# Expert tiles loaded one tile sooner, control numbers read later, the even tail put next to the loop

## The reference

```python
for s in range(S):
    fresh_e = int(np.argmax(logits[b, s]))
    if s == 0 or local_gate[b, s] < 0.5:
        e = fresh_e
    else:
        e = prev_e if prev_e >= 0 else fresh_e
    prev_e = e
    ...
    h = np.maximum(x[b, s] @ w1[e], 0.0)
    out[b, s] = p[e] * (h @ w2[e])
```

## Time and profile before

| | us |
|---|---|
| median of 3 runs | 699.01 |
| the runs | 695.54 to 708.86 |
| profiled execution, time | 697.34 |
| profiled execution, span | 695.5 |
| PE busy | 653.3 (94%) |
| VectorE busy | 319.5 (46%) |
| ScalarE busy | 207.7 (30%) |
| GpSimd busy | 213.2 (31%) |

### The profile page before, as it was taken

How to read it: one execution, slowest core, us unless ns; L and a number is a source line. 1 busy time by engine, 2 the same in 40 slices (tenths; PEclk the granted TensorE clock), 3 DMA queues, 4 the chain that set the end, 5 groups by cost and what they waited for, 6 DMA issues and landing times.

```text
span 695.5 us, 10536 instructions
## 1 busy us (share of the span) xinstructions
PE 653.3 (94%) x3370; PEld 530.5 (76%) x3371; DVE 319.5 (46%) x831; ACT 207.7 (30%) x410; POOL 213.2 (31%) x119
## 2 busy tenths in 40 slices
PE   8999999578989998999979989999999999999997
PEld 6777878456877787877767658888888888888886
DVE  4999787477435434534525775432231112311112
ACT  3666544204232332344202653132211112111110
POOL 0000002037567767799313745352000000000000
PEclk9999999879999999999999999999999999999999
DMA  8655356137447547578234322310010000000001
GB/s 304 249 208 177 115 172 247 43 122 257 155 161 261 182 167 256 180 221 283 90 139 121 91 91 91 122 61 1 1 60 1 1 0 1 30 32 1 0 1 60
DMA packets 35267, 82.66 MB, mean 119 GB/s; under 512 B 3347, under 2 KB 7699, under 8 KB 35221
## 3 DMA queue, kind: packets, MB, share of 16 engines
q1 hardware_dynamic: 17808, 40.20, 16.3%
q10 hardware_dynamic: 15492, 35.56, 15.5%
q0 software_dynamic: 1920, 6.29, 2.8%
HBM read 67.09 MB, written 14.94 MB: 118 GB/s over the span
## 4 chain that ended last, share of the span: by engine, by line
PE 76%; DVE 10%; DMA 7%; issue 4%; SPq 1%; ACT 1%; DVEq 0%; POOL 0%; ACTq 0%; POOLq 0%
PE psum L597 20%; PE psum L599 19%; PE psum L598 19%; DMA xs<-x_sorted 5%; PE psum L1886 5%; PE psum L1858 3%; PE psum L1869 2%; PE psum L1977 2%; PE psum L1796 1%; PE psum L1994 1%; PE psum L2037 1%; DVE prob L1405 1%; DMA bounds_i<-in_n_local 1%; DVE prob_t L1419 1%; DVE ys L1587 1%
## 5 line engine op out<-in xcount | busy, mean ns | idle before, releaser
L722 POOL TENSOR_TENSOR w<-raw,w 128x1024 fp32r<-128x1024 f32 x56 | 132.4, 2400 | 49.6 <-ACT w L820 49.6
L1750 DVE SCALAR_TENSOR_TENSOR act_t<-psum,act_t 128x512 fp32r<-128x512 f32 x48 | 33.2, 691 | 191.6 <-ACT act_t L1101 191.6
L820 ACT ACTIVATE w<-raw 128x1024 fp32r<-128x1024 f32 x64 | 67.4, 1058 | 132.9 <-PE psum L599 66.2
L1101 ACT ACTIVATE act_t<-psum 128x512 fp32r<-128x512 f32 x48 | 28.7, 598 | 217.8 <-PE psum L599 217.8
L597 PE MATMUL psum<-un_t,wc 128*128 128x512 f32 x192 | 75.3, 392 | 1.4 <-DVE un_t L1674 1.4
L597 PE MATMUL psum<-wc,act_t 128*128 128x512 f32 x192 | 75.6, 394 | 0.0
L598 PE MATMUL psum<-un_t,wc 128*128 128x512 f32 x192 | 75.4, 393 | 0.0
L599 PE MATMUL psum<-un_t,wc 128*128 128x512 f32 x192 | 75.4, 393 | 0.0
L599 PE MATMUL psum<-wc,act_t 128*128 128x512 f32 x192 | 74.8, 390 | 0.0
L598 PE MATMUL psum<-wc,act_t 128*128 128x512 f32 x192 | 74.8, 389 | 0.0
L874 ACT ACTIVATE prob<-prob,top 128x256 f32<-128x256 f32 (+1 forms) x96 | 46.3, 482 | 48.1 <-DVE top L1405 47.7
(11 more groups left out here) (271 smaller groups left out, 1111.3 us busy)
## 6 DMA issues: line engine op xcount, KB each, us to landing
raw<-in_moe_w ACTq DMA_DIRECT2D x60, 512.0 KB, 4.1
k_win<-in_k SPq DMA_DIRECT2D x8, 768.0 KB, 5.8
raw<-in_moe_w_ch SPq DMA_DIRECT2D x12, 512.0 KB, 3.3
v_win<-in_v SPq DMA_DIRECT2D x8, 704.0 KB, 4.6
xs<-x_sorted SPq DMA_DIRECT2D x16, 256.0 KB, 3.9
y_sorted<-ys SPq DMA_DIRECT2D x16, 256.0 KB, 2.6
q_t<-in_q SPq DMA_DIRECT2D x8, 384.0 KB, 3.4
out<-u SPq DMA_DIRECT2D x12, 256.0 KB, 2.0
```

The source lines that it names most:

```text
L722: nc.gpsimd.tensor_tensor(w[:, slot, 1, m, at_:at_ + PIECE], raw[:, n % RING, :], w[:, slot, 0, m, at_:at_ + PIECE].bitcast(f32), ALU.subt ...
L820: nc.scalar.activation(w[:, slot, 0, m, at_:at_ + PIECE], raw[:, n % RING, :], ACT.Copy).then_inc(high_done, 1)
L1101: nc.scalar.activation(act_t[n % 2][:, 0, :], bank(act_bank(n)), ACT.Relu).then_inc(act_high, 1)
L1750: nc.vector.scalar_tensor_tensor(act_t[n % 2][:, 1, :], bank(act_bank(n)), 0.0, act_t[n % 2][:, 0, :].bitcast(f32), ALU.max, ALU.subtract) ...
```

## The change

1. SyncE loads tile j+3 in step j into the other buffer, once PE has turned tile j+1. Tile 2 is asked for ahead of the loop as soon as tile 0 is turned. One tile beyond the even end is loaded and not used; ScalarE waits for it before it overwrites the region. GpSimd clears the end of `ctl` that this load's row number may be read from.
2. On PE, `place_of` is split into `ready_of` and `slot_of`. The slot of tile j+1 is read behind the transposes of hid(j), slot and readiness of tile j behind the transposes of the new tile, just ahead of the down product. The readiness of tile j+1, which wasn't used there, is not read.
3. On PE, the even tail stands in the If and the odd one in the Else. On SyncE, both share the two last steps.
4. At the start of the stage PE starts tile 0's up product before it turns tile 1, and VectorE does `share(1)` and `first_results` before tile 1's parts.
5. In the routing, the one-hot is held by expert, then tile, so that counts come out of PE in the order of the running sum. The copies `totals` and `ahead` go, for the second batch the copy of the counts as well (its counts are read from PSUM), and `area` and `count` are computed behind the slots.
6. `BANK_LAST` moves to bank 0, and four tiles' last gate sums stand before the last value product instead of two in the step before.

```diff
--- before.py
+++ after.py
@@ -232,10 +232,9 @@
     ends = rr("ends", [1, 2 * ST])
     counted = rr("counted", [P, 2 * ST * E])
     carry = rr("carry", [1, ST + 1])
-    one_hot = [rr(f"one_hot{b}", [P, ST, E]) for b in range(B)]
-    totals = rr("totals", [P, E, ST])
+    hot = [rr(f"hot{b}", [P, E, ST]) for b in range(B)]
+    one_hot = [x[:, :, :].rearrange("p e t -> p t e") for x in hot]
     upto = [rr(f"upto{b}", [P, E, ST]) for b in range(B)]
-    ahead = rr("ahead", [P, E, ST])
     area = rr("area", [P, E])
     rank = keep("rank", [P, ST, E])
     slot_f = rr("slot_f", [P, NT])
@@ -554,8 +553,9 @@
 
         small = bank(6)
         OVER = P + D
-        BANK_LOGITS, BANK_LAST, BANK_PART = (small[:, P + OVER + n * ST * (E + 1):P + OVER + (n + 1) * ST * (E + 1)]
-                                             for n in range(3))
+        BANK_LOGITS, BANK_PART = (small[:, P + OVER + n * ST * (E + 1):P + OVER + (n + 1) * ST * (E + 1)]
+                                  for n in range(2))
+        BANK_LAST = bank(0)[:, 0:ST * (E + 1)]
         BANK_FLAGS = small[0:ST, 2 * P:4 * P]
         BANK_KEEP, BANK_FRESH = small[0:ST, 2 * P:3 * P], small[0:ST, 3 * P:4 * P]
         BANK_ENDS = small[0:1, OVER:OVER + 2 * ST]
@@ -668,33 +668,32 @@
             sp.wait_ge(scattered, 16 * NT)
             for par in range(2):
                 load_tile(first_rows[par], par)
+            sp.wait_ge(xs_turned, 1)
+            load_tile(row_of(2), 0)
             sp.wait_ge(ctl_ready, 1)
             half = HALVES_LEAST + nc.sync.value_load(ctl[0:1, CTL_MORE], min_val=0, max_val=SLOTS // 2 - HALVES_LEAST)
             odd = nc.sync.value_load(ctl[0:1, CTL_ODD], min_val=0, max_val=1)
 
-            def tile_step(p, par, ahead):
+            def tile_step(p, par, loads):
 
                 j = 2 * p + par
-                if ahead >= 2:
-                    sp.wait_ge(xs_turned, j + 1)
-                    load_tile(row_of(j + 2), par)
+                if loads:
+                    sp.wait_ge(xs_turned, j + 2)
+                    load_tile(row_of(j + 3), 1 - par)
                 sp.wait_ge(ys_ready, j + 1)
                 sp.dma_start(y_sorted[ds(j * P, P), :], ys[par][:, :]).then_inc(ys_stored[par], 16)
 
             with sp.Fori(0, HALVES_LEAST - 1) as p:
-                tile_step(p, 0, 2)
-                tile_step(p, 1, 2)
+                tile_step(p, 0, True)
+                tile_step(p, 1, True)
             with sp.Fori(HALVES_LEAST - 1, SLOTS // 2 - 1) as p:
                 with nc.sync.If(half > p + 1):
-                    tile_step(p, 0, 2)
-                    tile_step(p, 1, 2)
+                    tile_step(p, 0, True)
+                    tile_step(p, 1, True)
+            tile_step(half - 1, 0, False)
+            tile_step(half - 1, 1, False)
             with nc.sync.If(odd > 0):
-                tile_step(half - 1, 0, 2)
-                tile_step(half - 1, 1, 1)
-                tile_step(half, 0, 0)
-            with nc.sync.Else():
-                tile_step(half - 1, 0, 1)
-                tile_step(half - 1, 1, 0)
+                tile_step(half, 0, False)
 
 
             for n in range(RING, 2 * FF // 256):
@@ -711,6 +710,7 @@
             nc.gpsimd.memset(ones[:, :], 1.0).then_inc(ones_ready, 1)
             for r in range(2):
                 nc.gpsimd.memset(v_flat[r][:, (2 * ST - 1) * P:], 0.0).then_inc(v_padded, 1)
+            nc.gpsimd.memset(ctl[:, CTL_ROW.stop:], 0)
             nc.gpsimd.memset(zeros[:, :], 0.0).then_inc(zeros_ready, 1)
             nc.gpsimd.memset(eps[:, :], LN_EPS).then_inc(eps_ready, 1)
 
@@ -1051,6 +1051,7 @@
             act.wait_ge(eps_ready, 1)
             scale_near(0, 0)
             scale_near(0, 1)
+            act.wait_ge(xs_loaded[0], 16 * half + 16)
             x2_part(0, 0)
             with nc.scalar.If(odd > 0):
                 last_result(2 * half + 1, 0, half)
@@ -1257,30 +1258,31 @@
             def take_counts(b):
 
                 dve.wait_ge(ranks_ready, b + 1)
-                link(nc.vector.tensor_copy(counted[:, :], BANK_COUNTED))
+                if b == 0:
+                    link(nc.vector.tensor_copy(counted[:, :], BANK_COUNTED))
 
             def rank_all(b):
-                flat_ = lambda x: x[:, :, :].rearrange("p a n -> p (a n)")
-                link(nc.vector.tensor_copy(totals[:, :, :], counted[:, ST * E:].rearrange("p (t e) -> p e t", t=ST)))
-                link(nc.vector.tensor_tensor_scan(flat_(upto[b]), row["run"], flat_(totals), 0.0, ALU.mult, ALU.add))
-                if b == B - 1:
-
-                    link(nc.vector.tensor_tensor(count[:, :], upto[0][:, :, ST - 1], upto[1][:, :, ST - 1], ALU.add))
-                link(nc.vector.tensor_tensor(ahead[:, :, :], upto[b][:, :, :], totals[:, :, :], ALU.subtract))
-                start = row["area"]
-                if b == 1:
-                    link(nc.vector.tensor_tensor(area[:, :], row["area"], upto[0][:, :, ST - 1], ALU.add))
-                    start = area[:, :]
-                link(nc.vector.tensor_tensor(ahead[:, :, :], ahead[:, :, :],
-                                             start.unsqueeze(2).broadcast_to([P, E, ST]), ALU.add))
-                link(nc.vector.tensor_tensor(rank[:, :, :], counted[:, 0:ST * E].rearrange("p (t e) -> p t e", t=ST),
-                                             ahead[:, :, :].rearrange("p e t -> p t e"), ALU.add))
+                by_tile = lambda x: x.rearrange("p (e t) -> p t e", t=ST)
+                sums_ = counted[:, :] if b == 0 else BANK_COUNTED
+                inside, totals = sums_[:, 0:ST * E], sums_[:, ST * E:]
+                start = row["area"] if b == 0 else area[:, :]
+                link(nc.vector.tensor_tensor_scan(upto[b][:, :, :].rearrange("p e t -> p (e t)"), row["run"], totals,
+                                                  0.0, ALU.mult, ALU.add))
+                link(nc.vector.tensor_tensor(rank[:, :, :], by_tile(inside),
+                                             start.unsqueeze(1).broadcast_to([P, ST, E]), ALU.add))
+                link(nc.vector.tensor_tensor(rank[:, :, :], rank[:, :, :],
+                                             upto[b][:, :, :].rearrange("p e t -> p t e"), ALU.add))
+                link(nc.vector.tensor_tensor(rank[:, :, :], rank[:, :, :], by_tile(totals), ALU.subtract))
 
             def place(b):
                 link(nc.vector.tensor_tensor(rank[:, :, :], rank[:, :, :], one_hot[b][:, :, :], ALU.mult))
                 link(nc.vector.tensor_reduce(slot_f[:, b * ST:(b + 1) * ST], rank[:, :, :], AX.X, ALU.add))
                 these = slice(b * ST, (b + 1) * ST)
                 nc.vector.tensor_copy(slots[:, these], slot_f[:, these]).then_inc(slots_ready, 1)
+                if b == 0:
+                    link(nc.vector.tensor_tensor(area[:, :], row["area"], upto[0][:, :, ST - 1], ALU.add))
+                else:
+                    link(nc.vector.tensor_tensor(count[:, :], upto[0][:, :, ST - 1], upto[1][:, :, ST - 1], ALU.add))
 
             def place_results():
 
@@ -1589,9 +1591,9 @@
                     rectify(j + 1, 1 - par, 1)
 
             x_tile(0, 0)
-            x_tile(1, 1)
             share(1)
             first_results()
+            x_tile(1, 1)
             rectify(0, 0, 0)
             rectify(0, 0, 1)
             tile_step(0, 0, 2)
@@ -1838,9 +1840,9 @@
             def rank_tokens(b):
 
                 pe.wait_ge(one_hot_ready, b + 1)
-                hot = one_hot[b][:, :, :].rearrange("p t e -> p (t e)")
-                nc.tensor.matmul(BANK_RANKS, before, hot, start=True, stop=True)
-                nc.tensor.matmul(BANK_TOTALS, ones[:, :], hot, start=True, stop=True).then_inc(ranks_ready, 1)
+                flags = hot[b][:, :, :].rearrange("p e t -> p (e t)")
+                nc.tensor.matmul(BANK_RANKS, before, flags, start=True, stop=True)
+                nc.tensor.matmul(BANK_TOTALS, ones[:, :], flags, start=True, stop=True).then_inc(ranks_ready, 1)
 
             with nc.tensor.If(windowed > 0):
 
@@ -1911,14 +1913,14 @@
                         tasks.append(lambda t=PART_STEP[n]: sum_part(t))
                     if n in THIRD_STEP:
                         tasks.append(lambda t=THIRD_STEP[n]: sum_third(t))
-                    if n == LAST_STEP:
-                        tasks += [lambda t=t: sum_last(t) for t in range(2)]
                     if n > 0:
                         values(n - 1, tasks)
+                for t in range(4):
+                    sum_last(t)
                 values(UNITS - 1)
                 pe.wait_ge(x_unit_done, UNITS)
                 turn_x(len(X_FILLS) - 1)
-                for t in range(2, ST):
+                for t in range(4, ST):
                     sum_last(t)
             with nc.tensor.Else():
                 pe.sem_inc(g_x, 1)
@@ -1994,11 +1996,11 @@
                     ins = nc.tensor.transpose(bank(4)[:, c * P:(c + 1) * P], xs[par][:, c * P:(c + 1) * P], ident)
```

(34 more changed lines are left out.)

## The result

The changed kernel takes **677.31 us** (median of 4 runs, 676.39 to 679.46), the kernel before beside it 700.1 us (4 runs, 695.54 to 708.86): ratio 0.970, 95% interval 0.9643 to 0.9757. Run again beside the last experiment it took 677.43 us (6 runs), ratio 0.9651 (0.9609 to 0.9692). The forecast was 677 with 671 to 686. Of the profiled executions the changed one took 677.65 us (span 675.8) against 697.34 (695.5), which is 19.7 us less where the sum said 20.95. All ratios here leave out runs more than 1.5% above the fastest of their own kernel; the medians take all runs.

The account below looks back on a forecast made before the run. TensorE (PE) was taken as the bound, so gains had to come from its stalls; terms of 8.1 + 2.6 + 6.1 + 3.0 + 0.75 + 0.4 = 20.95 us off 697.34 gave 676.3, predicted as 677, range 671 to 686.

Parts of the forecast that it names:

- The sum: All gains over the whole kernel added up: 20.95 us, chance 0.55 that it holds as it stands.
- Load, 8.1: Expert stage: token tile loads asked one tile sooner end PE's waits before the tile's transposes, 8.1 us.
- Control reads, 2.6: Expert stage: control reads moved behind the transposes end four issue waits at the hidden transposes, 2.6 us.
- Rival (4): Reads moved between products are bare because PE's sequencer stops running ahead after a wait: 704 us, chance 0.03.
- Against: the covered reads of odd steps: Sign against bare moved reads: in odd steps four reads are covered by matmuls already queued, no stall.
- Tail, 6.1: Behind the last loop step: without reads and long jump, PE's stall before tile 14 and slow matmuls go, 6.1 us.
- Rival (2): The tail's stall is the loop's exit, not the long jump; 2 us or more stay, 679 to 681, chance 0.15.
- Start, 3.0: Start of expert stage: sooner up product, no ReLU wait, no issue wait at tile 0, together 3.0 us.
- Slots 0.75: Routing: fewer VectorE links from counts to slots; control numbers come 0.75 us sooner.
- end of attention 0.4: End of attention: two tiles' gate sums leave the path before the last but one value product, 0.4 us.
- Expert 7's weights: GpSimd's weight pieces for expert 7: slack falls from 2.4 to 0.3 us; nothing taken, up to 1 us kept.
- Rival (1): The weights or a half-bare read give back 2 to 5 us: 679 to 682, chance 0.15.

Follow-up runs that it names:

- the last experiment: Changed kernel with the four control reads back ahead of the hidden transposes and the odd tail back next to the loop: 686.31 us.
- the second profile: Profile of the changed kernel run once more, unchanged: 676.66 us in that profile, median 677.43 us.
- experiment 11: Changed kernel with four idle control-number reads more ahead of each down product: 696.34 us, ratio 0.9912.

## Why the prediction was right, and where it wasn't

**The sum** was right within 1.3 us, in the profiled execution and by the median. What failed in it is the step that treated the terms as additive.

**Load, 8.1.** The waits went as forecast. But it isn't the worth of this edit: alone it gives 9 us by its ratio (0.013 x 703) and takes with it the head stalls, and taken out of the finished change it costs some 30 (30.6 us in the expert stage of the profile, 36 by the medians of different groups), since the other half of the change leans on it.

**Control reads, 2.6: mis-attributed.** The step was "the other four waits give 1.9 + 4 x 0.16". Those four went with the load edit. The sentence "I take nothing, as odd steps hide four" looked at steps in which no wait stood right ahead of the reads. Rival (4) named the true mechanism, "because PE's sequencer no longer runs ahead of them once it has passed a wait", and gave it 0.03 because it asked whether it holds in every step, not where a wait would stand. It holds in the steps in which the sequencer had to stand at a load's wait, at 1.2 to 1.4 us where PE was seen idle and 0.6 to 1.3 where it wasn't, and the changed kernel has none of these since the load edit took them away. "Against: the covered reads of odd steps" failed for the same reason: those reads stood a whole down product behind the wait. What the moved reads do bring, given the load edit, is 4.3 us by the medians of two groups: in the profile 2.0 at the head behind expert 7's weights and 2.0 as the reads' part of the tail.

**Tail, 6.1.** Right in size: 4.67 us before tile 14 and 1.01 of slow matmuls behind it (1.7 less 0.3 forecast; the wait at 341.25 is 0.33 and, with the overlap, 0.49 us). The long jump was taken as the price "of that order" of 2.68; it is 2.5. But the term belongs to reads and jump together, and either alone would have left 1.8. Rival (2), the loop's exit alone, is excluded as the sole cause: exit and reads without the long jump leave 1.84, exit alone nothing.
The Trainium skill ("Runtime: NRT & Kernel Launch", Instruction fetch mechanics) says that a taken branch whose target is outside the fetched window stalls for a page; the 2.5 us agree with that. Its 2048 instructions of TensorE's memory would keep a jump over some 300 inside, and the tail put back (1.76) speaks against that, unless the window is smaller than the memory, as its next remark on two lines has it.

**Start, 3.0** (measured 2.77). Right against the profile, and short by some 5 us against the usual run of before. The rows showed two operations at 1.92 and 2.32 us beside GpSimd; that these are two only by luck, and up to five in other runs, was not asked. It is the likeliest reason why the medians gained 23 and 24 us where the profiled executions gained 19.7.

**Slots 0.75 and end of attention 0.4**: 0.97 together instead of 1.15. The sums gave 0.67 (logits at 131.31), the chain to the slots 0.92 (139.83), but the control numbers only 0.37 of it: 0.2 go to the count, as forecast, and the rest is lost since a few of VectorE's small steps before them took up to 0.24 longer (143.37: 0.40 instead of 0.16). Why isn't shown; the scatter runs beside them in both kernels.

**Expert 7's weights**: slack 0.3, taken as nothing, 1 us kept. At 311.03 it was overdrawn by 0.13; in the second profile by 1.15, 1.5 with the reads put back. Rival (1) is real and stayed under its 2 us. In the second profile GpSimd's wait for ScalarE at that place is 2.30 us instead of 0.99 (301.95 against 301.05), and ScalarE had waited 4.77 instead of 3.76 us for a load of weights; why that load came later stays open.

## What to carry to other kernels

The cover of something an engine's sequencer must do is what it has queued since the last wait that held it, and such a wait need not show as idle time of the engine: look when the load landed, not only for a bracket. So before a scalar read or a jump is put down as free or as a cost, look for the wait that stands ahead of it, and take the wait away first: moved behind a wait, two cheap reads a step made the kernel 18 us slower; with the wait gone, the same move gains up to 4.
Edits that share a cover or a wait have no prices of their own. Price them as a pair, and test both the edit alone and the whole without it: alone and put back, the load edit measured 9 and some 30 us.
A kernel whose runs spread by 2% while another's spread by 0.5% may have a race for a resource in it, and one profile then shows one draw of it; several profiles, each taken of a slightly different kernel, showed 0.7 to 6.7 us for the same wait.

## What the runs showed of the hardware that I hadn't expected

- Single stalls of PE of 1.76 to 1.89 us left its clock alone (1.06 us for the eight transposes behind those at the tail). Above that the length alone does not decide: 2.17 us (load alone, 324.35), 2.43 (tail alone, 206.37), 2.73 and all from 4.26 to 6.68 lowered it to half, 2.41 (experiment 11, 358.56) and 2.71 (moved reads, 382.74) didn't. Of two stalls with only four transposes between them, 2.06 and 1.40, 0.98 and 1.18, 0.74 and 1.30 lowered it, 1.00 and 1.26 didn't. Where it fell, up to twelve products ran 0.43 us apart instead of 0.23, some 1 to 2 us more. It makes double stalls dearer than their brackets: 38 matmuls in the moved reads alone.
- A small VectorE operation in SBUF (2 to 768 numbers, twice 128x48) takes 1.9 to 2.4 us instead of 0.17 to 0.21 when it falls beside GpSimd's subtraction of 128x1024 tiles (2.36 us each), at most about the whole length of one such operation. Not each one does: L1308 (ten numbers) kept its 0.34 for two beside them. The casts and ReLUs of 128x512 out of PSUM beside the same subtractions stay at 0.69.
- A jump of PE over the odd branch costs 2.5 us of its sequencer, a read of a control number 0.67 to 0.70 (two of them 1.35 to 1.41 us in all fourteen profiles).
